# Attention and two feed-forward layers on one core: q and k handed over features first, without their transposes, with maxima and a second copy placed by DMA

## What is computed

```python
q_rot, k_rot = rotate(q), rotate(k)              # 4 batches x 8 heads, 576 positions, 64 features, fp32
scores = q_rot @ k_rot.T / 8                     # for each of the 32 heads
attn = softmax(scores, axis=-1)
x = (attn @ v) as [2304 tokens, 512]
x = (h - tanh(h)) @ w_out1,  h = x @ w_in1       # 512 -> 2048 -> 512
out = (h * sigmoid(1.702 h)) @ w_out2,  h = x @ w_in2
```

## Time and profile before

| | us |
|---|---|
| median of 3 runs | 1189.93 (1188.15 to 1190.78) |
| profiled execution, its own time | 1188.3 |
| its span, first to last instruction | 1186.5 |
| PE busy (matmuls) | 1146.3 |
| DVE, ACT, POOL busy | 471.2, 465.6, 188.9 |
| first S matmul with maxima (L503) | 21.62 |
| first stage-two matmul | 376.15 |

### The profile page before, as it was taken

One profiled execution on the slowest core, in us unless ns is written; L12 is line 12 of the kernel. 1 busy time (PEld: TensorE's weight loads), 2 busy tenths in 40 slices (PEclk: granted clock), 3 DMA queues, 4 the chain that ended last, 5 costly groups with the idle time before them and its releaser, 6 DMA issues.

```text
span 1186.5 us, 15852 instructions
## 1 busy us (share of the span) xinstructions
PE 1146.3 (97%) x6320; PEld 1051.4 (89%) x6320; DVE 471.2 (40%) x769; ACT 465.6 (39%) x811; POOL 188.9 (16%) x162
## 2 busy tenths in 40 slices
PE   5999999999999999999999999999999999999998
PEld 4788788777778999999999999999999999999997
DVE  6445545555553642333332323446332232323222
ACT  3655655665655532323222222345322222223222
POOL 6346545646501100000000000000000000000000
PEclk9999999999999999999999999999999999999999
DMA  4233344333321520000000000044000001000101
GB/s 112 51 86 79 78 117 138 86 101 91 104 64 56 186 81 27 27 28 27 27 28 27 1 28 27 27 134 133 27 27 22 5 27 28 27 27 1 27 1 27
DMA packets 78920, 65.79 MB, mean 55 GB/s; under 512 B 32256, under 2 KB 66048, under 8 KB 78848
## 3 DMA queue, kind: packets, MB, share of 16 engines
q1 hardware_dynamic: 78848, 64.79, 19.0%
HBM read 45.74 MB, written 14.23 MB: 51 GB/s over the span
## 4 chain that ended last, share of the span: by engine, by line
PE 89%; ACT 4%; DVE 4%; issue 2%; ACTq 0%; DVEq 0%
PE PS L556 34%; PE PS L574 17%; PE PS L571 17%; PE PS L515 10%; PE PS L500 4%; PE PS L503 3%; PE PS L478 3%; ACT k_hl L627 2%; ACT q_hh L633 1%; DVE q_lm L773 1%; DVE k_hl L768 1%; PE PS L467 1%; PE PS L487 1%; ACT q_lm L620 1%; DVE neg_max L762 1%
## 5 line engine op out<-in xcount | busy, mean ns | idle before, releaser
L556 PE MATMUL PS<-x_hi,w_parts 128*128 128x384 f32 x1536 | 423.1, 336 | 0.0
L556 PEld LDWEIGHTS PS<-x_hi,w_parts 128*128 128x128 f32 x1536 | 280.4, 188 | 4.3
L817 DVE TENSOR_TENSOR g_raw<-PS,act_t 128x384 f32<-128x384 f32 x192 | 107.1, 558 | 403.4 <-ACT act_t L688 202.7
L556 PE MATMUL PS<-x_lo,w_parts 128*128 128x384 f32 x768 | 257.2, 335 | 0.0
L571 PE MATMUL PS<-g_hi,w_parts 128*128 128x384 f32 x768 | 210.3, 334 | 0.8 <-DVE g_lo L822 0.8
L574 PE MATMUL PS<-w_parts,g_hi 128*128 128x512 f32 x576 | 195.1, 393 | 1.0 <-DVE y_sb L831 0.8
L515 PE MATMUL PS<-probs,v_one 128*128 128x288 f32 x640 | 181.7, 406 | 0.3 <-ACT pv_sb L616 0.3
L822 DVE TENSOR_TENSOR g_lo<-g_raw,g_hi 128x384 fp32r<-128x384 f32 x192 | 107.3, 559 | 113.6 <-ACT g_hi L695 113.6
L608 ACT ACTIVATE probs<-PS 128x576 f32<-128x576 f32 x160 | 104.2, 651 | 118.6 <-PE PS L503 113.8
L695 ACT ACTIVATE g_hi<-g_raw 128x384 fp32r<-128x384 f32 x192 | 100.8, 525 | 122.5 <-DVE g_raw L817 119.4
L762 DVE TENSOR_REDUCE neg_max<-PS 128x1 f32<-128x576 f32 x160 | 117.7, 754 | 76.9 <-PE PS L478 75.8
(11 more groups left out here) (64 smaller groups left out, 908.2 us busy)
## 6 DMA issues: line engine op xcount, KB each, us to landing
x_raw<-x_scratch SPq DMA_DIRECT2D x12, 768.0 KB, 4.5
raw_w<-moe_w_in_dram SPq DMA_DIRECT2D x32, 256.0 KB, 3.2
raw_w<-moe_w_out_dram SPq DMA_DIRECT2D x32, 256.0 KB, 3.4
k_h<-k_hl SPq DMA_DIRECT2D x16, 288.0 KB, 3.4
inv_wide<-inv_scratch SPq DMA_DIRECT2D x32, 144.0 KB, 3.0
x_scratch<-x_out SPq DMA_DIRECT2D x16, 288.0 KB, 2.4
x_scratch<-y_sb SPq DMA_DIRECT2D x6, 768.0 KB, 3.5
raw_k<-k_dram SPq DMA_DIRECT2D x16, 256.0 KB, 3.1
```

The costliest lines, as they stand in the source:

```text
L556: last = nc.tensor.matmul(h_banks[j % 2], w_parts[j][:, w, c * P:(c + 1) * P], x[par][:, c, :], start=(c == 0 and w == 0 and x is x_hi), s ...
L817: nc.vector.tensor_tensor(g_raw[:, j % 2, :], h_banks[j % 2], act_t[:, j % 2, :], ALU.subtract if m == 0 else ALU.mult).then_inc(g_done, 1)
```

## The change

q and k reach the kernel as [batch, head, feature, position]. `load` brings a pair of heads as 128 rows of 576 (`raw`) and again with the halves of the features swapped, in four transfers of 32 rows (`turned`): ten transfers for a pair, where there were four. The rotation is then three whole-tile operations. K and Q and their transposes are gone; ACT and DVE cut high and low parts from SBUF, three heads ahead (`PREPARED`), into four buffers. The queries' high part is cut once and copied to the other 64 partitions by a DMA (`copy_q`); keys are copied per head. The maxima of a head, [128, 5], are turned over by one transpose, ACT copies five rows to `max_rows`, and two DMAs lay them out as one row of `q_max` (`place_maxima`). `scores` waits for this row (`row_in`) before its second product. The inverse's store and its spreading are two places of SP's list. The output is in order, so a tile is stored by one DMA.

```diff
...
@@ -50,49 +51,21 @@
         for t in range(TILES):
             if now:
                 order.append(("S", h, t))
-            if ahead and t < TILES - 1:
-                order.append(("M", h + 1, t))
-                if t == TILES - 2:
-                    order.append(("M", h + 1, t + 1))
-        if h % 2 == 0 and h + 2 < NHEADS:
-            order.append(("K", h + 2, 0))
-        if ahead:
-            order.append(("R", h + 1, 0))
+            if ahead and t < 2:
+                order += [("M", h + 1, 2 * t + 1), ("M", h + 1, 2 * t + 2)]
+            if ahead and t == 2:
+                order.append(("R", h + 1, 0))
         if h + 2 < NHEADS:
-            order.append(("Q", h + 2, 0))
+            order.append(("M", h + 2, 0))
     return order
...
-    q_d, k_d, v_d = (t.rearrange("b h s d -> (b h) s d") for t in (q, k, v))
+    q_d, k_d = (t.rearrange("b h d s -> (b h d) s") for t in (q, k))
+    v_d = v.rearrange("b h s d -> (b h) s d")
...
             def load(t, src, pair):
-                par = pair % 2
-                heads = src[2 * pair:2 * pair + 2, :, :]
-                sp.dma_start(raw[t][par][:, :, 0:FULL, :],
-                             heads[:, 0:FULL * P, :].rearrange("a (p i) d -> p a (i d)", i=FULL)).then_inc(loaded[t][par], 16)
-                sp.dma_start(raw[t][par][0:TAIL, :, FULL, :],
-                             heads[:, FULL * P:SEQ, :].rearrange("a p d -> p a d")).then_inc(loaded[t][par], 16)
+                par, first = pair % 2, pair * P
+                sp.dma_start(raw[t][par][:, :], src[first:first + P, :]).then_inc(loaded[t][par], 16)
+                for b in range(P // 32):
+                    to, of = slice(32 * b, 32 * b + 32), first + 32 * (b ^ 1)
+                    sp.dma_start(turned[t][par][to, :], src[of:of + 32, :]).then_inc(loaded[t][par], 16)
...
-            def copy_k(pair):
-                par = pair % 2
-                sp.wait_ge(k_hi_done, 2 * pair + 2)
-                sp.dma_start(k_h1[par][0:HD, :, 0:SEQ].bitcast(F32), k_hl[par][0:HD, :, 0:SEQ].bitcast(F32)).then_inc(k_copied[par], 16)
+            def copy_k(h):
+                sp.wait_ge(k_hi_done, h + 1)
+                sp.dma_start(k_one[h % 4][own(h % 2), 0:SEQ].bitcast(F32), k_hl[h % 4][own(h % 2), 0:SEQ].bitcast(F32)).then_inc(k_copied[h % 4], 16)
+
+            def copy_q(h):
+                sp.wait_ge(q_hi_done, h + 1)
+                sp.dma_start(q_hh[h % 4][other(h % 2), 0:SEQ].bitcast(F32), q_hh[h % 4][own(h % 2), 0:SEQ].bitcast(F32)).then_inc(q_copied[h % 4], 16)
+
+            def place_maxima(h):
+                row = q_max[h % 4][one_row(h % 2), :].bitcast(F32)
+                sp.wait_ge(row_done, h + 1)
+                sp.dma_start(row[:, 0:FULL * P].rearrange("o (t n) -> o t n", t=FULL),
+                             max_rows[h % 2][0:FULL, :].bitcast(F32)).then_inc(row_in[h % 4], 16)
+                sp.dma_start(row[:, FULL * P:SEQ], max_rows[h % 2][FULL:TILES, 0:TAIL].bitcast(F32)).then_inc(row_in[h % 4], 16)
...
+            def store_inverse(pair):
+                sp.wait_ge(inv_done, pair + 1)
+                sp.dma_start(inv_scratch[pair].rearrange("a (p j) -> (a p) j", j=SEQ // HD), sums[pair % 2][:, :]).then_inc(inv_out, 16)
...
+            for h in range(2):
+                copy_k(h)
+                copy_q(h)
+            for h in range(-1, NHEADS):
+                pair = (h + 1) // 2
+                if h % 2 and pair + 2 < PAIRS:
+                    sp.wait_ge(k_lo_done, 2 * pair + 2)
+                    load("k", k_d, pair + 2)
+                    sp.wait_ge(q_lo_done, 2 * pair + 2)
+                    load("q", q_d, pair + 2)
+                if h % 2 and h >= 3:
+                    spread_inverse(h // 2 - 1)
+                if h >= 4 and h % 2 == 0:
+                    store_x(h // 2 - 2)
+                if h >= 1:
                     fetch_sums(h - 1)
-                    if pair:
-                        spread_inverse(pair - 1)
+                if h >= 0 and h % 2 == 0 and h // 2 + 1 < PAIRS:
+                    load_v(h // 2 + 1)
+                if h + 1 < NHEADS:
+                    place_maxima(h + 1)
+                if h + PREPARED < NHEADS:
+                    copy_k(h + PREPARED)
+                    copy_q(h + PREPARED)
+                if h >= 2 and h % 2 == 0:
+                    store_inverse(h // 2 - 1)
...
+                par, at = pair % 2, ((pair - 1) * 2 + "kq".index(t)) * 2 + 1
+                pool.wait_ge(loaded[t][par], (pair // 2 + 1) * 80)
+                nc.gpsimd.tensor_tensor(turned[t][par][:, :], turned[t][par][:, :], sin_sb[:, :], ALU.mult).then_inc(pool_chain, 1)
+                nc.gpsimd.tensor_tensor(raw[t][par][:, :], raw[t][par][:, :], cos_sb[:, :], ALU.mult).then_inc(pool_chain, 1)
+                pool.wait_ge(pool_chain, at + 2)
+                nc.gpsimd.tensor_tensor(raw[t][par][:, :], raw[t][par][:, :], turned[t][par][:, :],
+                                        ALU.add).then_inc(k_roped if t == "k" else q_roped, 1)
...
-                    pe.wait_ge(q_hi_done, 2 * h + 2)
+                    pe.wait_ge(q_copied[h % 4], h // 4 * 16 + 16)
...
-                for i in range(TILES):
-                    last = nc.tensor.transpose(slot[0:1, i * P:(i + 1) * P], neg_max[h % 2][:, i:i + 1], ident[:, :])
-                last.then_inc(r_ready, 1)
+                nc.tensor.transpose(slot_of("R", h)[0:TILES, 0, 0:P], neg_max[h % 2][:, :], ident[:, :]).then_inc(r_ready, 1)
...
+                    pe.wait_ge(k_copied[h % 4], h // 4 * 16 + 16)
...
+                    pe.wait_ge(row_in[h % 4], h // 4 * 32 + 32)
...
-                    if ahead and t in (2, 3):
-                        near_scores(h + 1, t)
-                    if ahead and t == 3:
-                        near_scores(h + 1, 4)
-                    if t == 4 and h % 2 == 0 and h + 2 < NHEADS:
-                        keys_across((h + 2) // 2)
-                    if t == 4 and ahead:
-                        maxima_across(h + 1)
                     if now and g >= 0:
                         probs_v(g)
-                    if ahead and t in (0, 1):
-                        near_scores(h + 1, t)
+                    if ahead and t < 2:
+                        near_scores(h + 1, 2 * t + 1)
+                        near_scores(h + 1, 2 * t + 2)
+                    if ahead and t == 2:
+                        maxima_across(h + 1)
                 if h + 2 < NHEADS:
-                    queries_across(h + 2)
+                    near_scores(h + 2, 0)
...
             def row(h):
                 act.wait_ge(r_ready, h + 1)
-                nc.scalar.activation(q_lm[h % 2][HD:HD + 1, :], slot_columns(slot_of("R", h), SEQ)[0:1], ACT.Copy).then_inc(row_done, 1)
+                if h >= 2:
+                    act.wait_ge(row_in[(h - 2) % 4], (h - 2) // 4 * 32 + 32)
+                nc.scalar.activation(max_rows[h % 2][0:TILES, :], slot_of("R", h)[0:TILES, 0, 0:P], ACT.Copy).then_inc(row_done, 1)
 
             def keys_hi(h):
-                act.wait_ge(kt_ready, h // 2 + 1)
+                if h < 2:
+                    act.wait_ge(first_roped, 1)
+                else:
+                    act.wait_ge(k_roped, h // 2)
                 if h >= 4:
-                    act.wait_ge(k_copied[h // 2 % 2], h // 4 * 16)
-                a = h % 2
-                nc.scalar.activation(k_hl[h // 2 % 2][0:HD, a, 0:SEQ],
-                                     slot_columns(slot_of("K", h - a), SEQ)[a * HD:(a + 1) * HD], ACT.Copy).then_inc(k_hi_done, 1)
+                    act.wait_ge(k_copied[h % 4], h // 4 * 16)
+                nc.scalar.activation(k_hl[h % 4][own(h % 2), 0:SEQ], raw["k"][h // 2 % 2][own(h % 2), :], ACT.Copy).then_inc(k_hi_done, 1)
 
...
             def queries_hi(h):
-                act.wait_ge(qt_ready, h + 1)
-                for rows in (slice(0, HD), slice(HD, P)):
-                    nc.scalar.activation(q_hh[h % 2][rows, 0:SEQ], slot_columns(slot_of("Q", h), SEQ)[0:HD], ACT.Copy,
-                                         scale=HD ** -0.5).then_inc(q_hi_done, 1)
+                if h < 2:
+                    act.wait_ge(first_roped, 2)
+                else:
+                    act.wait_ge(q_roped, h // 2)
+                if h >= 4:
+                    act.wait_ge(q_copied[h % 4], h // 4 * 16)
+                nc.scalar.activation(q_hh[h % 4][own(h % 2), 0:SEQ], raw["q"][h // 2 % 2][own(h % 2), :], ACT.Copy,
+                                     scale=HD ** -0.5).then_inc(q_hi_done, 1)
...
+            act.wait_ge(pads_set, 1)
+            for h in range(-PREPARED, NHEADS):
                 for t in range(TILES):
                     if h >= 0:
                         exp(h, t)
                     if t == 1 and h >= 1:
                         copy_pv(h - 1)
+                    if t == 2 and 0 <= h + 1 < NHEADS:
+                        row(h + 1)
                     if t == 2 and h in early_x:
```

(39 more changed lines are left out.)

244 lines of the change are left out of this document (78 added, 166 removed).

## The result

The changed kernel took 1199.97 us (median of 4 runs, 1197.33 to 1200.76) against 1189.87 (4 runs, 1188.15 to 1190.78): a ratio of 1.0083, 95% interval 1.0063 to 1.0102. It is slower, where a small gain was predicted. Its profiled execution took 1200.76 with a span of 1198.9, 12.4 more than the span in the earlier trace rows.

What follows compares the result with a forecast made beforehand. SP's transfer list, delaying the row of maxima at even heads, was taken as the bound. Start +6, pairs 1 to 12 -1.7, head 14 +6, other pairs -10.6, head 30 -1.8, end -1.8: -3.9, 1184.4, predicted 1186 us, range 1163 to 1208.

Steps and rivals of the forecast that it cites:

- the wait for K and Q is replaced by a wait for the row of maxima at even heads: Stage one, second half of S0: PE waits about 3 to 4 us at even heads of pairs 1 to 12.
- Head 30 and the end: Head 30, half a pair, gains 1.8 us; three stores for six at the end gain 1.8 us.
- narrow issues that are not near 0.6: SP's 32-row loads were priced at 0.60 us behind a narrow one; another price would show the prediction wrong.
- the period of 22.1: Pairs 1 to 12: S0 of head h+2 starts 22.1 us after S0 of head h, against 22.24 before.
- pairs 1 to 12: -1.7: Heads 2 to 25, where the inverse's store meets the ten loads: 12 x (22.1 - 22.24) = -1.7 us.
- the rival with cheap narrow transfers: Same chain on SP with narrow transfers at 0.43 us: period 20.7, time 1166 us; chance 0.22.
- The weights and the x load: Head 14's eight weight loads ahead of the ten loads, and the x load at head 12: +6 us, once.
- the low part 0.75: DVE's low part of the queries, in the chain to the row of maxima, takes 0.75 us, 9.0 to 9.8.
- The start: Before head 0: SP issues 26 transfers before the first copies; second placing lands at 27.5 against 21.62, +6 us.
- Pairs 0, 13 and 14: No meeting of the inverse's store and the ten loads: 3 x (18.7 - 22.24) = -10.6 us.
- Late maxima: The placing lands in 3.0 to 3.4 us: period 23.3 to 23.7, 1203 us; chance 0.34 including a held SP.
- PE as the bound: Issuing does not matter: twelve more pairs at 18.7 us, 1143 us with the start; chance 0.07.

Runs made afterwards that it cites:

- the filled waits: Changed kernel with the first half of S0 of even heads 4 to 26 computed nine times over, ahead of the wait for the maxima: 1196.76 us, ratio 1.0053.
- the version with the inverse in between: Changed kernel with the store of the inverse issued between the loads of k and q instead of ahead of both: 1179.45 us, ratio 0.9913.
- The late POOL: Changed kernel with POOL's rotation of pair 1 started only after DVE made the low part of head 1's queries: 1197.24 us, ratio 1.0072.
- v's loads: Changed kernel with inverse stored between k and q loads, weight loads spread, POOL's first rotation late, v's loads behind the placing: 1212.85 us, ratio 1.0198.
- the version without their move and without POOL's late start: Changed kernel with the inverse stored between the loads of k and q and head 14's weight loads spread over four heads: 1169.53 us, ratio 0.9831.

## Why the prediction was wrong

**Right.** The bound that takes over: "the wait for K and Q is replaced by a wait for the row of maxima at even heads", and the chain that makes it, link by link. PE alone needs 9.0 us a head (heads 27 and 29, with no wait at their end, took 9.05 and 9.02). L231 lands 1.8 us after its issue (113.53 to 115.35). Copies cost nothing after the first. Head 30 and the end gave 1.8 and 1.9. The largest wait is at head 16. Its own sign of being wrong, narrow issues that are not near 0.6, is what the trace showed first.

**The step that failed** is the period of 22.1 with its sum, "pairs 1 to 12: -1.7", and in it the clock: the sum adds what PE waits and puts what comes behind a wait at nothing. By the links it should have been 22.1 - 1.25 = 20.85, since ten loads took 4.7 and not 5.95 (the price of the rival with cheap narrow transfers was right, its time was not). It was 23.3 in the mean. That the forecast was off by 14 us only is luck, since two large errors have opposite signs. Over pairs 1 to 12, from the predicted +4.3 to the measured +10.1:
- Narrow loads cheaper: 12 x 1.25, -15.0.
- The lower clock behind the waits, which the prediction did not have at all. The row of maxima of an odd head is ready 5.97 us after its even head's start at full clock and near 7.56 in a head with such a stretch, 8.3 in heads 14 and 16. Four heads with 1.6 and two with 2.35: +11.1, an estimate from these rows. The pairs with a stretch took 1.5 more than those without, and the filled waits took 1.6 to 2.1 out of each of five heads; the 2.35 of heads 14 and 16 they did not take out.
- The weights and the x load: head 15 took 18.85 and head 13 14.69 against some 11.4, 10.7 for the predicted 6: +4.7. Moving them shows it: the weights brought 4 on the changed kernel and 10 on the version with the inverse in between, and with the x load moved as well heads 12 to 15 took 4.6 less.
- Low parts at up to 1.86 for 0.75, through the inverse (12.26 for 11.4 in head 6), an issue of v that held SP 0.7 to 1.0 longer in two pairs, and what isn't told apart: +7.3. This is a remainder; heads 6 and 7 close without the rest, 22.1 - 1.25 + 0.86 = 21.71, as measured.
- The period before was 22.43 in the mean of 12 pairs, not the 22.24 of the one that was read: -2.3.

The price of the low part, "the low part 0.75", was read from the group in which one operand came from PSUM; the change takes both from SBUF, beside a busy POOL. The prediction did not use a rule that bears on this: the Trainium skill, "SBUF — State Buffer", section "SBUF: two separate sides", has VectorE and GpSimd share one port pair, locked for the whole instruction against a VectorE operation with two SBUF inputs. The trace agrees in part: 1.84 for 0.75 on DVE and none on the row maxima from PSUM (0.75 beside the rotation), and POOL's own operations grew too, 1.41 to 1.9. But strict turns of 0.75 and 1.41 would take 2.16 us, and at the start one operation of each took 1.8 to 1.9.

**The start**, +9.2 for +6: six operations of DVE at 1.1 more each on the way to head 0 are 6.6, less what 26 issues cost less than 0.61 each. The late POOL gave 5.5 of it back. **Pairs 0, 13 and 14**, -3.3 for -10.6: "18.7 for a pair without the loads" held for single heads (9.05), but head 26 took 11.32 with the lower clock behind its wait, head 28 13.79 with the wait of 2.38 for DVE and the lower clock behind it, and pair 0 took 19.83.

**The rivals.** Late maxima is where the time fell, and its direction was right; its mechanism was not, for the landing was 1.8, not 3, except behind large transfers at heads 14 and 16 (3.9 and 4.2). PE as the bound was refuted. What the prediction cited of one wide transfer (the Trainium skill, "DMA: Bandwidth & Descriptors", section "Rules for kernel authors") agrees on issues: the narrow ones cost 2.8 us of SP a pair.

## What to carry to other kernels

When one queue issues everything, a transfer's price is what stands behind it in the list, and moving one gives at one place and takes at another: look at both places, the one that it leaves and the one that it enters (v's loads: 1212.9, where the version without their move and without POOL's late start, which by itself cost nothing, had 1169.5; the store of the inverse, which left five loads free to go ahead, was worth 20). Read a price from a row with the same operand memories and the same neighbour at work, not from the same operation. And add to each new wait of TensorE what it costs afterwards, since the work behind it may run at the lower clock.
